# Eight array tiles over two PSUM banks for parts of a delta-rule chain, and its grams and products in another place of a step

## What is computed

```python
for t in range(S):                                   # attention, per batch and head
    kt, vt, bt = (k_n[:, :, t], v[:, :, t], beta[:, :, t, None])
    y[:, :, t] = np.einsum('bhd,bhde->bhe', q[:, :, t], state)
    v_old = np.einsum('bhde,bhd->bhe', state, kt)
    state = state + bt[:, :, :, None] * np.einsum('bhd,bhe->bhde', kt, vt - v_old)
h = x @ w_in                                         # first layer
g = np.where(h >= 1, h, np.where(h <= -1, 0.0, (h + 1) ** 2 / 4)); x = g @ w_out
r = np.maximum(x @ w_in2, 0.0)                       # second layer
return (r * r) @ w_out2
```

## Time and profile before

| what | value |
|---|---|
| median of three runs | 1000.12 us (1000.01 to 1000.48) |
| the profiled execution, its own time | 1000.15 us |
| its span in the trace | 998.2 us |
| PE busy | 981.7 us, 98% |
| DVE busy | 583.1 us, 58% |
| ACT busy | 419.2 us, 42% |

### The profile page before, as it was taken

The page is one execution under the profiler, slowest core; times in us unless marked ns, Lnnn a source line. Parts: engine busy times, 40 slices in busy tenths (PEclk is TensorE's granted clock), DMA queues, the critical chain, the costliest instruction groups (busy, mean ns, idle before and its releaser), DMA issues.

```text
span 998.2 us, 24906 instructions
## 1 busy us (share of the span) xinstructions
PE 981.7 (98%) x10566; PEld 804.3 (81%) x10566; DVE 583.1 (58%) x1465; ACT 419.2 (42%) x749; POOL 25.4 (3%) x34
## 2 busy tenths in 40 slices
PE   6899999999999999999999999999999999999998
PEld 6578788888888888888888888888888888888887
DVE  7769878776877687769535774433434334334332
ACT  4777544433434434424445553333333233333332
POOL 2510000000000000000000000000000000000000
PEclk9889999999999999999999999999999999999999
DMA  6342232003200410020003411001010010000000
GB/s 217 97 160 72 69 97 77 10 18 94 76 10 18 114 56 18 18 65 33 2 12 128 158 64 64 1 1 64 0 64 1 1 64 1 27 6 1 32 1 32
DMA packets 28413, 50.97 MB, mean 51 GB/s; under 512 B 2320, under 2 KB 15760, under 8 KB 28304
## 3 DMA queue, kind: packets, MB, share of 16 engines
q1 hardware_dynamic: 28304, 49.39, 15.3%
HBM read 39.94 MB, written 9.44 MB: 49 GB/s over the span
## 4 chain that ended last, share of the span: by engine, by line
PE 96%; ACT 2%; issue 1%; DMA 1%; DVE 0%; SPq 0%; DVEq 0%; ACTq 0%
PE psum L1120 40%; PE psum L1096 39%; PE psum L903 3%; PE psum L880 2%; PE psum L972 2%; PE psum L920 2%; PE psum L856 1%; PE psum L1009 1%; PE psum L929 1%; PE psum L1017 1%; PE psum L1040 1%; PE psum L1004 1%; ACT ring L622 1%; PE psum L1013 0%; DMA kt_sb<-in_k_t 0%
## 5 line engine op out<-in xcount | busy, mean ns | idle before, releaser
L1120 PE MATMUL psum<-g_hi,w 128*128 128x512 f32 x1152 | 392.1, 395 | 0.1
L1096 PE MATMUL psum<-x_hi,w 128*128 128x512 f32 x1152 | 387.0, 390 | 0.0
L1382 DVE TENSOR_TENSOR g_lo<-act_g,g_hi 128x512 fp32r<-128x512 f32 x192 | 132.6, 691 | 214.5 <-ACT g_hi L746 214.3
L1120 PEld LDWEIGHTS psum<-g_hi,w 128*128 128x128 f32 x1152 | 216.1, 188 | 50.8 <-issue 2.0
L1096 PEld LDWEIGHTS psum<-x_hi,w 128*128 128x128 f32 x1152 | 216.2, 188 | 45.6 <-issue 0.2
L746 ACT ACTIVATE g_hi<-act_g 128x512 fp32r<-128x512 f32 x192 | 121.4, 632 | 273.3 <-PE psum L1120 239.4
L1120 PE MATMUL psum<-g_lo,w 128*128 128x512 f32 x576 | 224.6, 390 | 0.0
L1096 PE MATMUL psum<-x_lo,w 128*128 128x512 f32 x576 | 224.1, 389 | 0.0
L1376 DVE TENSOR_TENSOR act_g<-act_g 128x512 f32<-128x512 f32 x96 | 66.4, 692 | 112.9 <-ACT act_g L739 112.9
L1096 PEld LDWEIGHTS psum<-x_lo,w 128*128 128x128 f32 x576 | 108.1, 188 | 22.4 <-issue 0.2
L1120 PEld LDWEIGHTS psum<-g_lo,w 128*128 128x128 f32 x576 | 108.2, 188 | 20.6
(11 more groups left out here) (101 smaller groups left out, 607.5 us busy)
## 6 DMA issues: line engine op xcount, KB each, us to landing
kt_sb<-in_k_t SPq DMA_DIRECT2D x24, 256.0 KB, 4.0
qt_sb<-in_q_t SPq DMA_DIRECT2D x24, 256.0 KB, 3.6
kn_sb<-in_k_n SPq DMA_DIRECT2D x20, 256.0 KB, 4.1
ring<-in_v_s SPq DMA_DIRECT2D x24, 192.0 KB, 2.7
between_layers<-y_out SPq DMA_DIRECT2D x6, 768.0 KB, 5.1
x_sb<-between_layers SPq DMA_DIRECT2D x6, 768.0 KB, 5.7
result<-y_out SPq DMA_DIRECT2D x5, 768.0 KB, 3.9
wi_st<-in_w_in SPq DMA_DIRECT2D x7, 384.0 KB, 3.1
```

What stands on the lines that cost most here:

```text
L1096: ins = pe.matmul(h_ps[n % 2][:, :], w_in_part(layer, f // GW, part)[:, kt, fs], x[:, kt, :], start=(kt == 0 and j == 0), stop=(kt == KT - ...
L1120: ins = pe.matmul(acc[kt][:, :], w_out_part(layer, f // GW, part)[:, f % GW, ds], g[n % 2][:, :], start=(f == 0 and j == 0), stop=(f == NF ...
L1382: dve.tensor_tensor(g_lo[n % 2][:, :], act_g[n % 2][:, :], g_hi[n % 2][:, :].bitcast(F32), ALU.subtract).then_inc(g_lo_ready, 1)
```

## The change

- A second bank for the chain in tiles 1 to 4 (chunks 2 to 5): `both_ps` is banks 6 and 7. Even and odd heads of a pair use different rows of the array (state part) or are crossed over to the columns of the neighbouring batch (solve), so that eight tiles of the array are in use. The state part has 32 products of 48 columns in place of 16 of 96. The gram part keeps its 32 products, head halves one after the other. Tile 0 keeps the old forms (`substitute_first`, and the branch `n == 1` of `solve`).
- `u_sb` is laid out so that ACT's copy can take two batches' heads of one row block from both banks (`u_pair`, `by_pair`); the number of copies and their size stay.
- `diagonals_of(n)` takes both halves at once, 128 products with the halves alternating, in step 4 (5 in tile 0).
- Grams of chunk n go to steps 0 to 3 of its tile; none is made a chunk ahead, but for chunk 1.
- In tiles 1 to 4, steps 0 to 12, `blocks` (diagonals, grams, keys by queries) stand behind the step's second product; the chain stays between the products.
- Waits for the shared banks: solve and substitute of blocks 1 and 2 wait for masks (`kq_ready`), keys by queries for residuals (`r_ready`) and for the copies of `solved` (`u_ready`).
- DVE: `residual` right behind `clamp`, `masked` behind `g_low`. ACT: the square behind `solved`.

```diff
+        both_ps = psum[:, 6:8, :]
+        def u_pair(b, a):
+            return b // 2 * 2 * HP + 2 * a + b % 2
+        def solve_group(b, hp):
+            return b - b % 2 + (hp + b) % 2
         def gram_at(t, f):
-            at = ({0: 1, 1: 2, 2: 3}, {4: 1, 5: 2, 6: 3}, {5: 2, 6: 3})[min(t, 2)]
-            ahead = {11: 0, 12: 1} if t else {12: 0}
...
+            at = {b: b for b in range(B)} if t else {0: 1, 1: 2, 2: 3}
+            return B * (t + 1) + at[f] if f in at and t + 1 < NC else None
         def diagonal_at(t, f):
-            at = f - (4 if t == 0 else 1)
-            return (t + 2, at // 2) if t + 2 < NC and at in (0, 2) else (None, None)
+            return t + 2 if t + 2 < NC and f == (4 if t else 5) else None
+        def behind_second(t, f):
+            return t > 0 and f < 13
...
-                square_part(n)
+                if not t:
+                    square_part(n)
                 k = solve_at(t, f)
                 if k is not None:
                     for b in range(B):
                         solved(k, b)
+                if t:
+                    square_part(n)
...
                 for i in range(NB):
                     for a in range(HP):
                         for b in range(B):
-                            k = kt_sb[hp * DP:hp * DP + D, (B * n + b) % KEYS, a, block_rows(i)]
...
+                            for hp in range(2):
+                                k = kt_sb[hp * DP:hp * DP + D, (B * n + b) % KEYS, a, block_rows(i)]
+                                ins = pe.matmul(gd_ps(n, hp)[block_rows(b), (i * HP + a) * BLK:(i * HP + a + 1) * BLK], k, k,
+                                                start=True, stop=True)
                 ins.then_inc(gd_done, 1)
...
+                    if n > 1:
+                        pe.wait_ge(r_ready, NB * (n - 1) + 2)
...
+                    if n > 1 and b == 1:
+                        pe.wait_ge(u_ready, B * (NB * (n - 1) + 2))
+                    elif n > 1:
+                        pe.wait_ge(r_ready, NB * (n - 1) + 3)
...
+                if i == 2:
+                    pe.wait_ge(kq_ready, 2 * (B * n + 2))
+                pe.wait_ge(state_ready, 4 * n)
+                for a in range(HP):
+                    for hp in range(2):
+                        for b in range(B):
+                            rows = slice(hp * DP, hp * DP + D)
+                            ins = pe.matmul(both_ps[block_rows(b), hp, a * D:(a + 1) * D],
+                                            kt_sb[rows, (B * n + b) % KEYS, a, block_rows(i)], s_bd[rows, b * HP + a, hp, :],
+                                            start=(a == 0), stop=(i == 0 and a == HP - 1))
...
+                if n > 1 and i in (1, 2):
+                    pe.wait_ge(kq_ready, 2 * (B * n + (1, 3)[i - 1]))
...
+                for a in range(HP):
                     for b in range(B):
...
+                        for hp in range(2):
+                            j = 2 * a + hp
+                            ins = pe.matmul(both_ps[block_rows(solve_group(b, hp)), b % 2, a * D:(a + 1) * D],
+                                            xc[block_rows(b), place(i, j), :], ring[block_rows(b), k % RING, j, :],
+                                            start=True, stop=True)
...
+            def beside(t, f):
+                of_chain(t, f)
+                if not behind_second(t, f):
+                    blocks(t, f)
...
+                if behind_second(t, f):
+                    blocks(t, f)
...
+                k = residual_at(t, f)
+                if k is not None and t:
+                    residual(k)
                 if split_at(n):
                     split_weights(*split_at(n))
                 ahead(t, f, False)
                 activated(n)
-                k = residual_at(t, f)
-                if k is not None and t:
-                    residual(k)
                 m = products_at(t, f)
-                if m is not None:
+                if m is not None and not behind_second(t, f):
                     masked(m)
                 ahead(t, f, True)
...
                 g_low(n)
+                if m is not None and behind_second(t, f):
+                    masked(m)
```

More of the change, by code:

```diff
@@ L297, in half_heads, with u_pairs, u_of, by_pair @@
             return slice(part * HH, (part + 1) * HH)
+        def u_pair(b, a):
+            return b // 2 * 2 * HP + 2 * a + b % 2
+        def u_pairs(b, first=0, past=HP):
+            return slice(u_pair(b, first), u_pair(b, past - 1) + 1, 2)
         def half_pairs(b, part):
[L300 to L305, removed]
+            return u_pairs(b, part * HP // 2, (part + 1) * HP // 2)
+        def u_of(b, j, rows):
+            at = j % 2 * HW
+            return u_sb[0:rows, u_pair(b, j // 2), at:at + D]
+        def solve_group(b, hp):
+            return b - b % 2 + (hp + b) % 2
+        def by_pair(ps):
+            return ps[:, :, 0:HP * D].rearrange("p h (a e) -> p a h e", e=D)
         def solve_at(t, f):
@@ L930, in substitute @@
                                             gram[b][0:i * BLK, place(0, j), (i - 1) * BLK:i * BLK],
-                                            u_of(b * H + j, i * BLK), start=False, stop=(j == H - 1))
+                                            u_of(b, j, i * BLK), start=False, stop=(j == H - 1))
                             if j == H - 1:
                                 ins.then_inc(s_done, 1)
+            def substitute(k):
+                n, i = divmod(k, NB)
+                if n == 1:
+                    return substitute_first(k)
+                pe.wait_ge(u_ready, B * (k - NB))
+                pe.wait_ge(gram_ready, 2 * B * (n + 1))
+                pe.wait_ge(gd_ready, 2 * min(n + 1, NC - 1))
+                if i == 2:
[8 more added lines that the diff above has]
+                                            start=(a == 0), stop=(i == 0 and a == HP - 1))
+                            if i == 0 and a == HP - 1 and hp:
+                                ins.then_inc(s_done, 1)
+                if i == 2:
+                    ins.then_inc(odd_state_part, 1)
+                if i:
+                    for hp in range(2):
+                        if i == 2 and hp:
+                            pe.wait_ge(odd_state_part, n - 1)
+                        for a in range(HP):
+                            for b in range(B):
+                                j = 2 * a + hp
+                                ins = pe.matmul(both_ps[block_rows(b), hp, a * D:(a + 1) * D],
+                                                gram[b][0:i * BLK, place(0, j), (i - 1) * BLK:i * BLK],
+                                                u_of(b, j, i * BLK), start=False, stop=(a == HP - 1))
+                                if a == HP - 1 and hp:
+                                    ins.then_inc(s_done, 1)
             def first_substitute(k, part):
@@ L987, in outputs @@
                     pe.wait_ge(kq_plain, 2 * B)
-                elif b < 2 and c + 1 < NC:
-                    pe.wait_ge(gram_ready, 2 * (B * (c + 1) + (2 if c > 1 else 1)))
                 elif b > 1:
@@ L1040, in state_change, with of_chain @@
                         ins = pe.matmul(ds_ps[hp * DP:(hp + 1) * DP, at:at + D], kn_sb[:, m % 2, 2 * a + hp, :],
[L1041 removed]
+                                        u_of(b, 2 * a + hp, P), start=True, stop=True)
                 ins.then_inc(ds_done, 1)
[L1044 removed]
+            def of_chain(t, f):
                 k = residual_at(t, f)
@@ L1130, in _ @@
                 gram_of(m)
-            for hp in range(2):
-                diagonals_of(1, hp)
+            diagonals_of(1)
             for m in range(B):
```

86 lines of the change are left out of this document (47 added, 39 removed).

## The result

The changed kernel takes **1023.3 us** (four executions, 1020.51 to 1025.26) where the kernel before takes 1000.07 (998.53 to 1000.48): a ratio of 1.0233 with a 95% interval of 1.0206 to 1.0260, so 2.3% slower. The forecast was 1009 with a range of 998 to 1018: the direction held, the size did not. The profiled execution is the fastest of the four, the one of 1020.51 us (span 1018.6).

A forecast was written before the change was run, and what follows sets the result against it. The prediction took TensorE (PE) to bound the kernel. From 1000.15 us, -10.4 for eight tiles, +5.2 interruptions, +4.6 mask waits and +9.5 dry running gave 1009 us, 0.9% slower, with a range of 998 to 1018.

The forecast's parts named there:

- What bounds the kernel: TensorE (PE), busy 98% of the span: each microsecond it saves or loses in tiles 0 to 4 is the run's.
- Part 1: Solve, state part and diagonal blocks: eight array tiles at 6.6 ns a record need less PE time, -10.4 us.
- Rival C: Small groups: eight tiles run no faster than four, gains shrink to 0.1 us, 1018 us; chance 0.07.
- Part 2: Moved groups in tiles 0 to 4: 23 more interruptions of wide matmuls at 0.23 us each, +5.2 us.
- Part 3: Steps 8 and 9, tiles 1 to 4: PE waits for DVE's masks because bank 7 is shared, +4.6 us.
- Part 4: Merged diagonal groups, tiles 0 to 3: PE runs out of instructions at ends of 256-instruction packets, +9.5 us.
- Rivals A and B: A: instructions come in time, 999.6 us, chance 0.13; B: masks come in time too, 995 us, chance 0.07.
- Rival D: Clock falls to 1.2 GHz behind a pause; one fall in wide work costs 6.8 us, 1016 us; chance 0.08.

## Why the prediction went wrong, step by step

- **What bounds the kernel** was right: every microsecond of PE came through. No wait was hidden and nothing was given back later.
- **Part 1, eight tiles, is the term that was mis-sized**: -10.4 forecast, -2.5 measured, 7.9 of the 11.5 us by which the profiled execution missed 1009. I took 6.6 ns a record from two records at the edge of a group, whose 0.01 us are within the rounding, and let it outweigh the 8.6 ns that 128 records in a row had shown in the same rows. Halving the columns brought four tiles and eight to the same 8.8 ns: a floor near this was in the diagonals' row all along. Rival C, with its 0.1 us of gain, was nearer on this term; I had given it 0.07.
- **Part 2, interruptions**, was right: 6.5 us (4.1 to 8.9) for 6.2 in a kernel that has little else. (23 x 0.23 is 5.3, not 5.2.)
- **Part 3, masks**, was right in size (4.5 us by the trace's waits for 4.6) and in both places: 0.4 in step 8, as forecast, and 0.7 to 0.8 in step 9 for 0.95. The path to step 9's wait, through the square behind the copies, was right. In step 8 the residual waited for PE's own substitute (0.16 us in tile 2), not for the late clamp; the two ends lie so close that the 0.4 came out by luck, and putting the square back did not take it away. What stands behind the waits was missed: a wait also holds the request for the next packet, which cost 2.2 us in tile 4.
- **Part 4, dry running**, was right in place to the instruction, and somewhat too long in size: 2.0 to 2.3 us in tiles 1 to 3 for 2.7, 1.0 behind tile 0's group for 1.4. Rivals A and B are ruled out by the experiments with the shifted count and with the group taken apart.
- **Rival D was part of the truth**: three falls of the clock, not one, and each of 1.1 to 1.5 us where I had priced 6.8 from the fall ahead of the loop. The forecast carried none of it, since it treated the fall as another case and not as a companion of the waits that it forecast itself.

With 2.5 for the gain, 4.6 for the slower wide work and 2.2 for tile 4 in their places, the forecast's own sum would have been 1023.7, less the 2.3 us ahead of the loop 1021.4; the execution took 1020.5.

What stays open: why the clock falls behind some waits of 2 us and not behind others. The length alone does not tell: a wait of 2.00 us (tile 3) had a fall behind it and one of 2.02 (tile 2) had none, and with four tiles one of 2.06 had it and one of 2.13 had none.

None of these kernels beats the one before; the nearest, four tiles with the new places, is 0.65% slower.

## What to carry to other kernels

Before spreading small matmuls over more of the array, divide the time of a long group by its records: where halving the columns would not shorten it, more tiles will not either; what is left is fewer instructions, which no run here tried. A run of small instructions without wide work between can stand still for 2 us when a packet's end falls some 300 instructions into it or later (302 did here, 272 did not); put a wide product in between, and count 256 to see where the ends fall. A wait on the busiest engine costs more than its length, since it can hold the next packet's request, and a standstill of 2 us can be followed by a slower clock.

## What the runs showed of the hardware that was not expected

- PE's start pace is about 8.5 to 8.8 ns for a load and a matmul together, with four tiles and with eight, at 32 and at 24 columns; 48 columns cost 9.5 ns with eight tiles and 10.8 with four.
- The request for a packet of 256 instructions can stand behind an unmet semaphore wait: in six cases the transfer began 1.30 to 1.36 us after the end of the masks that the wait was for, and PE ran dry for 1.3 to 2.1 us in all of them; with 64 instructions more ahead of it, one of these dry runs was gone.
- A standstill of some 2 us was followed by a clock of 0.50 for some 3 us in some places (0.52 on the mean of 3.3 us behind tile 4's) and by none in others.
